# First batch of a scan, MLP and expert attention kernel: the running products of two units summed on TensorE, one store and one load issued at other places

## The reference

```
scale = min(|a|, 0.999) / (|a| + 1e-6);  a_n = a * scale            # a = a_re + i a_im
for t in range(S):
    S_re, S_im = a_n[t] * S (complex) + (outer(k[t], v[t]), 0)
    y[t] = q[t] @ S_re
x = y of all heads side by side                                     # (B, S, 384)
h = relu(x @ w_in);  g = sigmoid(conv3(h));  x = (h * g) @ w_out    # 384 -> 1024 -> 384
for e in range(4):  out += gate_e * softmax_causal(x wq_e (x wk_e)^T / 8) (x wv_e) wo_e
```

## Time and profile before

| what | value |
|---|---|
| median of 3 runs | 755.3 us (755.08 to 756.08) |
| the profiled execution, whole | 751.82 us |
| its span | 749.8 us |
| PE busy | 662.7 us (88%) |
| DVE busy | 614.0 us (82%) |
| ACT busy | 410.4 us (55%) |
| first matmul on PE | 62.32 us |
| first matmul of the MLP of batch 0 | 122.45 us, its second half from 125.53 us |

### The profile page before, as it was taken

One profiled execution on the slowest core, in us unless ns is written; L12 is line 12 of the kernel. 1 busy time (PEld: TensorE's weight loads), 2 busy tenths in 40 slices (PEclk: granted clock), 3 DMA queues, 4 the chain that ended last, 5 costly groups with the idle time before them and its releaser, 6 DMA issues.

```text
span 749.8 us, 13183 instructions
## 1 busy us (share of the span) xinstructions
PE 662.7 (88%) x5226; PEld 501.4 (67%) x5226; DVE 614.0 (82%) x1165; ACT 410.4 (55%) x747; POOL 0.2 (0%) x4
## 2 busy tenths in 40 slices
PE   0006989999999999999999999999999999999998
PEld 0002768776666788776566788776566888998765
DVE  3999998999999787998989787998988675773663
ACT  6404367434667656335668647335667335654565
POOL 0000000000000000000000000000000000000000
PEclk9999999999999999999999999999999999999999
DMA  8704785200049464100058464100055440000001
GB/s 342 270 0 119 203 244 189 93 0 1 0 121 271 121 181 159 61 0 1 0 142 258 124 175 167 48 1 0 1 147 170 131 128 2 1 0 1 2 22 43
DMA packets 93628, 73.84 MB, mean 98 GB/s; under 512 B 8704, under 2 KB 85760, under 8 KB 92928
## 3 DMA queue, kind: packets, MB, share of 16 engines
q1 hardware_dynamic: 93568, 73.01, 32.1%
HBM read 49.34 MB, written 23.65 MB: 97 GB/s over the span
## 4 chain that ended last, share of the span: by engine, by line
PE 53%; DVE 32%; ACT 7%; issue 3%; DMA 3%; SPq 0%; DVEq 0%; ACTq 0%
DVE cv L1138 6%; PE wide L1603 6%; PE wide L1448 5%; PE wide L1584 5%; PE bank L1655 4%; PE wide L1639 4%; PE bank L1663 4%; PE wide L1460 3%; PE wide L1513 3%; DVE m L956 3%; PE wide L1534 3%; DVE heads L1143 3%; PE wide L1579 2%; DVE m L955 2%; PE wide L1575 2%
## 5 line engine op out<-in xcount | busy, mean ns | idle before, releaser
L1513 PE MATMUL wide<-x_hi_lo,win_hi 128*128 128x384 f32 x384 | 107.7, 350 | 3.4 <-DVE x_hi_lo L1102 2.6
L1513 PEld LDWEIGHTS wide<-x_hi_lo,win_hi 128*128 128x128 f32 x384 | 69.8, 188 | 7.7 <-issue 4.6
L1534 PE MATMUL wide<-heads,wout 128*128 128x384 f32 x200 | 70.1, 494 | 4.8 <-DVE heads L1143 4.8
L1202 DVE TENSOR_REDUCE nmax<-wide 128x1 f32<-128x768 f32 (+2 forms) x96 | 55.3, 618 | 21.1 <-PE wide L1613 21.0
L1138 DVE SCALAR_TENSOR_TENSOR cv<-h,wconv,cv 128x768 f32<-128x768 f32 x64 | 64.9, 1014 | 9.0 <-ACT cv L681 7.4
L1603 PE MATMUL wide<-attn 64*128 64x512 f32 (+3 forms) x256 | 65.0, 482 | 2.3 <-ACT attn L705 2.3
L1513 PE MATMUL wide<-x_hi_lo,win_lo 128*128 128x384 f32 x192 | 64.5, 336 | 0.0
L729 ACT ACTIVATE xs<-wide 128x896 f32<-128x896 f32 x48 | 44.1, 918 | 37.1 <-PE wide L1639 37.1
L655 ACT ACTIVATE h<-wide 128x384 f32<-128x384 f32 x64 | 29.6, 490 | 56.0 <-PE wide L1513 29.2
L1422 PE MATMUL wide<-attn,ident 128*128 128x512 f32 x4 | 3.9, 1082 | 62.3 <-ACT m L620 62.3
L1534 PEld LDWEIGHTS wide<-heads,wout 128*128 128x128 f32 x200 | 36.6, 189 | 30.5 <-DVE heads L1143 10.3
(11 more groups left out here) (205 smaller groups left out, 1505.1 us busy)
## 6 DMA issues: line engine op xcount, KB each, us to landing
heads<-heads_dram SPq DMA_DIRECT2D x96, 192.0 KB, 3.6
araw<-a_in SPq DMA_DIRECT2D x12, 768.0 KB, 6.2
araw<-qk_in SPq DMA_DIRECT2D x12, 768.0 KB, 4.7
heads_dram<-m SPq DMA_DIRECT2D x18, 384.0 KB, 3.6
heads_dram<-araw SPq DMA_DIRECT2D x18, 384.0 KB, 2.9
v<-v_in SPq DMA_DIRECT2D x4, 1536.0 KB, 6.7
out_dram<-h SPq DMA_DIRECT2D x24, 192.0 KB, 2.1
heads_dram<-m SPq DMA_DIRECT2D x12, 192.0 KB, 2.8
```

Of the source, the lines that this page charges most:

```text
L1202: dve.tensor_reduce(nmax[:, t, side:side + 1], slot_scores(t, side), AXX, ALU.max, negate=True).then_inc(s_nm, 1)
L1513: last = MM(low[u % 2][:, 0:NT], w[:, k, mt * P:(mt + 1) * P], xs[:, k, n * NT:(n + 1) * NT], start=(k == 0 and part == 0), stop=(k == KT ...
L1534: last = MM(mlp_bank[u][:, 0:NT], wout[:, mt, k * P:(k + 1) * P], hgate(mt)[:, n * NT:(n + 1) * NT], start=(mt == 0), stop=(mt == MT - 1))
```

## The change

It touches batch 0 alone (apart from one wait that is always satisfied later on).

- **Sums on TensorE.** For units 1 and 2 (`SUMMED`) DVE only makes the four products (`summed_product`), the fourth one into free space in `xs`. PE adds or subtracts them by matmuls with the identity or its negative into PSUM (`fill_sums`), and ACT copies the sums back into `w_re` and `w_im` (`fill_copy`). The sum of the squares of unit 1 is made by PE too (`w_sums`, 1536 columns), and Ln and the Newton step read it from PSUM (`w_total`).
- **PE begins earlier.** The matmuls of `w_in_rest` wait for the seventh of the ten steps, no longer for the first inverse. The sums and `w_sums` follow, and only then `keep_busy`.
- **DVE's order.** The products of unit 2 stand among the work of unit 0, and the decays behind the first chunk of unit 1.
- **SP's order.** `store_first_chunk(1)` (chunk 2) stands before the store and load of the decays, and `load_a(1, 0)` behind `load_heads` of chunk 3.
- **ACT's order.** The Exp tables and `ln(1, 0)` stand behind `copy_k` of chunk 4.

```
+        def fill_of(w, u):
+            return groups(w)[:, u * UNIT_RUNS:(u + 1) * UNIT_RUNS, 0:WITHIN, 1:GROUP]
@@ sync @@
             load_heads(0, 1)
+            store_first_chunk(1)
             store_decay(0)
             load_decay(0)
-            store_first_chunk(1)
             load_heads(0, 2)
             store_unit(0, 1)
-            load_a(1, 0)
@@ sync, main(b), behind load_heads(b, 3) @@
                 else:
+                    load_a(1, 0)
                     store_first_chunk(2)
                     load_a(1, 1)
@@ scalar @@
+            def fill_copy(u, part):
+                act.wait_ge(s_fm, 4 * (u - 1) + part + 3)
+                act.wait_ge(s_fs, 2 * (u - 1) + part + 1)
+                nc.scalar.activation(fill_of((w_re, w_im)[part], u),
+                                     fill_sum(part).rearrange("p n (i g) -> p n i g", g=WITHIN),
+                                     ACT.Copy).then_inc(s_fc, 1)
@@ scalar, main(0) @@
                         if c == 3:
+                            exp_tables()
+                            ln(1, 0)
                             guess(1, 0)
...
                         if c == 2:
                             magnitude(1, 1)
-                            exp_tables()
-                            ln(1, 0)
@@ vector @@
+            def summed_product(u, n):
+                if n == 0:
+                    dve.wait_ge(s_cum, cum_count(0, HEAD))
+                val, fac, temps = cum_fill(u)
+                by = ((w_re, w_re), (w_im, w_im), (w_re, w_im), (w_im, w_re))[n]
+                dst = temps[n] if n < 3 else fill_extra(u).rearrange(...)
+                TT(dst, val(by[0]), fac(by[1]), ALU.mult).then_inc(s_fm, 1)
@@ vector, before main @@
             cum(0, 0, HEAD + 1)
-            for u in range(2):
...
+            for n in range(3):
+                summed_product(1, n)
+            w_sumsq(0, 0)
+            summed_product(1, 3)
+            for n in range(2):
+                summed_product(2, n)
+            inverse(0, 0)
+            scale_qk(0, 0)
+            products_by_chunk(0, 0)
+            for n in range(2, 4):
+                summed_product(2, n)
+            products_by_chunk(0, 1)
+            inverse(0, 1)
+            scale_qk(0, 1)
+            dve.wait_ge(s_fc, 2)
+            products_by_chunk(1, 0)
+            decay(0)
+            w_sumsq(0, UNITS - 1)
+            mask(0, 0)
+            state_sum(0, 0)
+            products_by_chunk(1, 1)
@@ tensor @@
+            def fill_sums(u):
+                planes_of = ((m[:, 0, unit(u)], ident, m[:, 1, unit(u)], negated),
+                             (m[:, 2, unit(u)], ident, fill_extra(u), ident))
+                for part, (one, one_by, other, other_by) in enumerate(planes_of):
+                    pe.wait_ge(s_winl, part + 1)            # unit 1; for unit 2 the copies of unit 1
+                    pe.wait_ge(s_fm, 4 * (u - 1) + 2 * part + 2)
+                    for runs_of in (slice(0, GROUP), slice(GROUP, UNIT_RUNS)):
...
@@ tensor, before main @@
-            pe.wait_ge(s_r0, 1)
+            pe.wait_ge(s_cum, cum_count(0, WITHIN))
...
+            fill_sums(1)
+            w_sums()
+            fill_sums(2)
             keep_busy(HOLD)
-            pe.wait_ge(s_winl, 1)
+            pe.wait_ge(s_fc, 4)
```

More of the change, by code:

```diff
@@ L83 @@
 HOLD = 3
+SUMMED = (1, 2)
 LAST = B - 1
@@ L614, in w_ln @@
                 act.wait_ge(s_n, UNITS * b + u + 1)
-                nc.scalar.activation(m[:, 1, unit(u)], m[:, 0, unit(u)], ACT.Ln).then_inc(s_nl, 1)
+                nc.scalar.activation(m[:, 1, unit(u)], w_total(b, u), ACT.Ln).then_inc(s_nl, 1)
             def w_guess(b, u):
@@ L884, in _ @@
             nc.scalar.activation(negated[:], ident[:], ACT.Copy, scale=-1.0).then_inc(s_neg, 1)
+            w_in_low(0)
             w_squares(0, 0)
+            w_in_low(1)
             w_ln(0, 0)
             w_guess(0, 0)
+            w_in_low(2)
+            for part in range(2):
+                fill_copy(1, part)
             w_squares(0, 1)
-            w_in_low(0)
             w_ln(0, 1)
             w_guess(0, 1)
-            w_in_low(1)
-            w_in_low(2)
+            for part in range(2):
+                fill_copy(2, part)
+            w_squares(0, 2)
             copy_k(0, 0)
-            w_squares(0, 2)
             w_ln(0, 2)
@@ L1033, in inverse_first @@
             def inverse_first(b, u):
-                total, y0, t = (m[:, r, unit(u)] for r in range(3))
+                y0, t = (m[:, r, unit(u)] for r in (1, 2))
                 dve.wait_ge(s_r0, UNITS * b + u + 1)
-                TT(t, total, y0, ALU.mult).then_inc(s_rn, 1)
+                TT(t, w_total(b, u), y0, ALU.mult).then_inc(s_rn, 1)
             def inverse_second(b, u):
@@ L1424, in w_in_rest, with w_sums @@
                 last.then_inc(s_wrest, 1)
+            def fill_sums(u):
+                planes_of = ((m[:, 0, unit(u)], ident, m[:, 1, unit(u)], negated),
+                             (m[:, 2, unit(u)], ident, fill_extra(u), ident))
+                for part, (one, one_by, other, other_by) in enumerate(planes_of):
+                    if u == 1:
+                        pe.wait_ge(s_winl, part + 1)
+                    else:
+                        pe.wait_ge(s_fc, 2 * (u - 2) + part + 1)
+                    pe.wait_ge(s_fm, 4 * (u - 1) + 2 * part + 2)
+                    for runs_of in (slice(0, GROUP), slice(GROUP, UNIT_RUNS)):
+                        cols = slice(runs_of.start * fill_size, runs_of.stop * fill_size)
+                        MM(fill_sum(part)[:, runs_of, :], one_by[:], one[:, cols], start=True, stop=False)
+                        last = MM(fill_sum(part)[:, runs_of, :], other_by[:], other[:, cols], start=False, stop=True)
+                    last.then_inc(s_fs, 1)
+            def w_sums():
+                pe.wait_ge(s_winl, KT)
+                pe.wait_ge(s_wsq, SUMMED[0] + 1)
+                for cols in (slice(0, 512), slice(512, UC)):
+                    for r in range(2):
+                        last = MM(w_total(0, SUMMED[0])[:, cols], ident[:], m[:, r, unit(SUMMED[0])][:, cols],
+                                  start=r == 0, stop=r == 1)
+                last.then_inc(s_n, 1)
             def transpose_k(b, c, part):
```

38 lines of the change are left out of this document (20 added, 18 removed).

## The result

The changed kernel takes **759.46 us** (median of 20 runs, 755.85 to 763.85) against 755.12 for the kernel before beside it (20 runs): a ratio of 1.0063 (1.0046 to 1.0080). The forecast was 756.3, within 752.8 to 758.3. Twelve more runs on another chip gave 758.17, ratio 1.0042 (1.0013 to 1.0071). Over all runs of this study, 32 of the changed kernel have a mean of 759.3 and 177 of the kernel before one of 755.9, 3.5 us less (2.5 to 4.4, from resampling the runs). The profiled executions lie further apart, 761.15 and 751.82.

The account below looks back on a forecast made before the run. It took DVE to bound the start until 96 us and the DMA queue from about 93. PE's sums 0, DVE's saving 0 and the queue +1.0 took the median from 755.3 to 756.3 us, range 752.8 to 758.3.

Parts of the forecast that it names:

- DVE, PE, ACT up to the first chunk: Batch 0's start: unit 1's inverse 5.3 us earlier, chunk 4's products 2 to 3; new PE and ACT work costs 0.5.
- The queue, steps 1 to 4: SP's DMA queue up to chunk 3's loads: chunk 2's loads at 84.0 instead of 84.99, chunk 3's at 92.3 instead of 93.23.
- Step 5: SP's queue from chunk 3's loads: with the gates behind them, chunk 4's stores land at 102.6 instead of 101.6, 1.0 later.
- the gates' 2.4 us: Transfer of the next gates between chunk 3's loads and chunk 4's stores: 768 KB at some 330 GB/s, 2.4 us.
- the bounds: Ends for the transfers from chunk 3's loads to chunk 4's stores: from a gain of 1.4 us to 1.4 later, at 281 GB/s.
- The clock's rival: PE idles over 3 us before chunk 4 and falls to half clock: +1.2 above the forecast, 757.5 us; chance 0.28.
- I count a shift of this moment once, in full: Any shift of PE's start on the MLP's first block with the last chunk goes fully into the total, once.
- The base of 125.53: Time in the old profile when PE starts the MLP's first block with the last chunk; the shift is counted from it.
- DVE's gain is hidden behind the queue: DVE's 4.2 us less work in batch 0 counts 0, because chunk transfers wait for SP's DMA queue.

Follow-up runs that it names:

- after_again: The changed kernel unaltered, profiled and run once more on another chip: 758.17 us, ratio 1.0042 to the kernel before.
- gates_alone: The kernel before with only the load of unit 0's next gates moved behind chunk 3's loads: 757.99 us, ratio 1.0038.
- gates_behind_stores: The changed kernel with unit 0's next gates loaded one place later still, behind chunk 4's stores: 758.12 us, ratio 1.0031.
- seam_free: gates_back with ACT's squares of the next but one batch's unit 1 moved behind the next batch's copy_k: 752.02 us, repeated 752.38.
- gates_back: The changed kernel with the load of unit 0's next gates again ahead of chunk 3's loads: 754.24 us, repeated 757.58.
- clock_kept: The changed kernel with six more keep_busy matmuls on PE in the wait before chunk 4: 761.62 us, repeated 757.62.
- before_seam: The kernel before with only ACT's squares of the next but one batch's unit 1 moved behind the next batch's copy_k: 755.88 us, ratio 0.9995.
- before_again: The kernel before, unaltered, profiled a second time in one run: 759.80 us.
- seam_gates_late: The changed kernel, gates left late, with ACT's squares of the next but one batch's unit 1 behind the next batch's copy_k: 756.19 us, ratio 1.0016.
- hold_more: gates_back with six instead of three keep_busy matmuls on PE before the first chunk: 755.57 us, ratio 1.0008.

## Why the prediction was wrong

- *DVE, PE, ACT up to the first chunk*: right. Unit 1's inverse 71.58 (71.5 forecast), mask of chunk 1 at 84.16 (84.6), chunk 4's products at 90.64 (91 to 92).
- *The queue, steps 1 to 4*: right. Decays landed at 82.86 (83.1), chunk 2's loads went out at 83.73 (84.0), chunk 3's at 92.07 (92.3). That PE would wait 2.33 us for chunk 2 the sum didn't have.
- *Step 5* had the right mechanism and the wrong size; this is the step that failed. "Chunk 4's stores have landed at 102.6"; they landed at 104.8. From chunk 3's loads to that landing it took 12.7 us, where the sum had 8.0 + 2.3 = 10.3. Leg by leg: chunk 3 landed at 97.9, as the sum had it, and the stores landed 2.3 behind the gates, as it had them. **The term that was too small is the gates' 2.4 us; it measured 4.7**, and 4.9 in after_again. In the seven profiles with the gates between these loads and stores, it took 9.7 to 10.8 us from the issue of these loads to the landing of the gates, where the sum has 3.3 + 2.4 + 2.3 = 8.0, and the stores took 2.3 to 2.4 more.
- *Why the gates took that long* is in part open. Their term rested on the rate of a queue at work, some 330 GB/s. From 98 to 100 us it was 217, with the DMA engines as busy as at 350 before; no run says why. The emptied queue started slowly as well: in the first 3 us of chunk 3's loads it moved 87 to 158 GB/s in the eight profiles with nothing ahead of them, and 237 to 302 in six where the gates went ahead. One issue of these loads took 1.56 us in place of 0.47, but that is not bound to the empty queue: the four took 1.9 us in gates_alone and gates_behind_stores, and 2.7 in seam_free with the gates ahead. As chunk 3 still landed when forecast, this start doesn't explain the 2.3 us by itself. Nor is the landing set by the bytes ahead of it alone, as the sum had it: 0.7 MB of unit 1's gates had moved by then. The lowest rate in the bounds was 281 GB/s; 2.36 MB in 12.7 - 2.3 us are 227.
- *The place of the gates as the cause* is shown: with that one line undone the mean is that of before (gates_back), and the line alone makes the kernel before slower (gates_alone).
- The prediction took from the Trainium skill (DMA: Bandwidth & Descriptors, "Queues, rings and completion order"), where each DMA engine consumes an issuing engine's descriptors in order, that the stores can't pass the gates. The traces agree: in the changed kernel the stores waited behind them, and in gates_behind_stores it was the loads, 6.4 us to landing in place of 4.0.
- *The clock's rival* was the case that happened, and it was priced too low. It decided "from an idle of about 2 us"; the idle was 5.76. It counted one chunk's copy at half clock, +1.2. The clock stayed low for 17.1 us, 5.6 us by clock_kept. The profile was read right, but it has one such fall, of 3.4 us, and the prediction names no other length; in the three profiles with this order the fall lasted 17.1, 17.1 and 3.4 us.
- *"I count a shift of this moment once, in full"* failed in the other direction. In the profiles the second half moved by 7.9 us and the end by 9.5, but the runs differ by 3.5. The base of 125.53 was that of an execution fast by chance, 4.1 us below the mean, and the changed kernel's profile lies 1.8 above its own; another execution of the kernel before has 133.14. So in some executions part of what the late gates cost is being lost already.
- *"DVE's gain is hidden behind the queue"*: right in its outcome for the change with the gates in place (755.8 against 755.9 in the mean), open as to the reason. With ACT's squares moved in both kernels, the change with the gates in place is worth 2.6 us (1.0 to 4.2). That is 2.6 more than without the move (0.6 to 4.6). So a gain was there (of DVE's work and the early stores together) and did not reach the end. That it is held up in ACT's wait fits the profiles, in which this wait is gone. Why before_seam gains nothing is not shown: its one profile has the second half at 134.04 after 17.1 us of low clock, but that execution is the slowest of its twelve runs.

## What to carry to other kernels

A transfer that fills a wait can be nearly free, as the gates were in their old place. Behind the wait it cost 4.7 us in place of the 2.4 that its bytes gave at the queue's best rate, since what the next stage needs lands behind it. Before pricing a change in one profile's microseconds, compare its mean clock and its time with those of the runs: an execution that was fast by chance may name the wrong bound. When a gain on one engine doesn't show, look for an early, blocking instruction on another engine at the end of the loop, since moving that one may release it. Then compare with the old kernel with the same instruction moved.

## What the runs showed of the hardware

- The low clock lasts very differently after like causes: 3.4 us after 1.78 us of idle in the first profile of before, 13.7 after 1.40 in before_again, 17.1 after 2.14 in before_seam. After 4.44 us of idle in seam_gates_late it was 3.4 again. In the first three PE was busy throughout the low stretch (13.70 of 13.70 us in the row above). In the changed kernel six more matmuls in the wait of 5.8 us kept the clock full, twice.
- A load of 768 KB took 6.2 us to land in the wait before chunk 3's loads, 7.4 behind these loads, and 9.7 with another such load and a chunk's stores ahead of it. One DMA issue on SP usually takes about 0.5 us; some took 1.06 and 1.56, and one of a 768 KB load in clock_kept 2.81. At the same DMA share of 0.93 the queue moved 350 GB/s from 93 to 94 us in the kernel before and 217 from 98 to 100 us in the changed kernel.
- In the middle of batch 0, over 30 us, PE's work in the profiles of before and of hold_more agreed to 0.01 us when counted from the second half's start. The runs of one kernel still spread over 4 to 11 us; in the profiles that were compared the differences arose at a few waits, for DMAs above all, and in the clock behind them.
